# A three-stage network on one core: order of the second stage's vector work, the split of w_out2, and who copies the first block product out of PSUM

## The reference, cut to what matters

```python
# attention without softmax, 8 batches, 8 heads, seq 576, head size 64
kv = einsum('bhsd,bhse->bhde', k, v);  o = einsum('bhsd,bhde->bhse', q, kv)
x = o / sqrt(mean(o*o) + 1e-6) * g_norm                 # -> (8, 576, 512)
# first block
h = relu(x @ w_in);  u, v = h[..., :512], h[..., 512:]
v_n = (v - mean(v)) / sqrt(var(v) + 1e-6)
gated = u * (einsum('ts,bsd->btd', w_spatial, v_n) + b_spatial)
x = gated @ w_out
# second block
h = relu(x @ w_in2)                                      # (8, 576, 1024)
c = conv over seq, 3 taps per channel (conv_w), zero padding
out = (h * sigmoid(c)) @ w_out2                          # (8, 576, 512)
```

## Time and profile before

| | |
|---|---|
| median of 3 runs | 854.7 us |
| the profiled execution | 855.42 us, span 853.6 us, mean granted TensorE clock 0.992 |
| busy, share of span | PE 94%, PEld 82%, DVE 69%, ACT 49%, POOL 5% |
| phase 1, batch 3 | 47.04 us |
| phase 1, batches 1 and 2 together | 111.95 us |
| phase 2, an even and an odd batch | 49.25 and 55.15 us |

### The profile page before, as it was taken

One profiled execution on the slowest core, in us unless ns is written; L12 is line 12 of the kernel. 1 busy time (PEld: TensorE's weight loads), 2 busy tenths in 40 slices (PEclk: granted clock), 3 DMA queues, 4 the chain that ended last, 5 costly groups with the idle time before them and its releaser, 6 DMA issues. The chain is left out here.

```text
span 853.6 us, 15487 instructions
## 1 busy us (share of the span) xinstructions
PE 802.4 (94%) x5654; PEld 700.6 (82%) x5654; DVE 588.0 (69%) x1254; ACT 419.3 (49%) x753; POOL 40.1 (5%) x48
## 2 busy tenths in 40 slices
PE   8999969899999999999998998999899998998998
PEld 6679759598898979798996886978779687796976
DVE  3766555557667575758888788587876878669683
ACT  3664242433525262532636647365564555546563
POOL 4342020010000000000000000000000000000000
PEclk9999989989999999999999999999999999999999
DMA  9862615835435362222452120121210212102101
GB/s 311 276 230 57 238 76 169 298 86 223 148 98 182 78 240 70 83 57 98 164 228 98 50 95 31 35 97 50 98 50 12 97 49 97 49 13 97 49 1 61
DMA packets 35001, 96.86 MB, mean 113 GB/s; under 512 B 2738, under 2 KB 9106, under 8 KB 30228
## 3 DMA queue, kind: packets, MB, share of 16 engines
q1 hardware_dynamic: 33476, 90.09, 31.0%
q10 hardware_dynamic: 1488, 6.30, 2.0%
HBM read 66.11 MB, written 30.28 MB: 113 GB/s over the span
## 5 line engine op out<-in xcount | busy, mean ns | idle before, releaser
L627 PE MATMUL ps<-w_in_split,v_hg_split 128*128 128x512 f32 x832 | 209.6, 398 | 24.7 <-DVE v_hg_split L1295 17.4
L627 PEld LDWEIGHTS ps<-w_in_split,v_hg_split 128*128 128x128 f32 x832 | 151.4, 188 | 77.0 <-DVE v_hg_split L1295 38.9
L451 PE MATMUL ps<-w_sp_split,v_hg_split 128*128 128x288 f32 x896 | 120.4, 295 | 1.7 <-DVE w_sp_split L1121 1.3
L451 PEld LDWEIGHTS ps<-w_sp_split,v_hg_split 128*128 128x128 f32 x896 | 119.2, 188 | 2.1 <-issue 1.5
L451 PE MATMUL ps<-x_operand_split,w_in_split 128*128 128x288 f32 x768 | 105.5, 298 | 2.6 <-ACT work L709 2.6
L451 PEld LDWEIGHTS ps<-x_operand_split,w_in_split 128*128 128x128 f32 x768 | 103.1, 189 | 5.2 <-ACT work L709 3.3
L482 PE MATMUL ps<-w_in_split,x_operand_split 128*128 128x512 f32 x384 | 93.5, 396 | 0.0
L915 ACT ACTIVATE work<-work 128x576 f32<-128x576 f32 x64 | 44.0, 687 | 94.0 <-DVE work L1284 94.0
L482 PEld LDWEIGHTS ps<-w_in_split,x_operand_split 128*128 128x128 f32 x384 | 70.4, 188 | 20.9 <-issue 6.1
L1244 DVE TENSOR_TENSOR h_and_sums<-work,ps 128x288 f32<-128x288 f32 x64 | 27.5, 453 | 71.7 <-PE ps L619 39.4
L1244 DVE TENSOR_TENSOR h_and_sums<-h_and_sums,ps 128x288 f32<-128x288 f32 x160 | 67.1, 448 | 7.7 <-PE ps L619 7.4
(11 more groups left out here) (125 smaller groups left out, 1101.7 us busy)
## 6 DMA issues: line engine op xcount, KB each, us to landing
kv_raw<-kv_main_dram SPq DMA_DIRECT2D x8, 2048.0 KB, 10.2
q_raw<-q_T_dram SPq DMA_DIRECT2D x8, 1152.0 KB, 7.1
operand_scratch<-t_then_s SPq DMA_DIRECT2D x8, 1152.0 KB, 5.3
operand_raw<-operand_scratch SPq DMA_DIRECT2D x8, 1152.0 KB, 5.4
sq_then_r<-r_scratch SPq DMA_DIRECT2D x14, 576.0 KB, 6.0
operand_scratch<-work SPq DMA_DIRECT2D x24, 288.0 KB, 2.6
operand_more_raw<-operand_scratch SPq DMA_DIRECT2D x8, 864.0 KB, 7.1
w_out_split_scratch<-v_hg_split ACTq DMA_DIRECT2D x2, 2048.0 KB, 10.5
```

The costliest lines, as they stand in the source:

```text
L451: last = pe.matmul(pair[bank][:, c, :], st, mo[:, c * HALF:(c + 1) * HALF], start=(n == 0), stop=(n == len(steps) - 1))
L627: last = pe.matmul(PS[:, ROW_BANK[i], :], x, wout2[:, w, F_ORDER[e], :], start=(e == 0 and n == 0), stop=(e == FT - 1 and n == len(PASSES) ...
```

## The change

Five edits. (1) The storage order of the operand blocks is B11, B21, T2, T1, T3, T4, B22, so T1 comes with the first load. (2) The subtractions for w_out2 go from GpSimd to VectorE (`wo2_low`), and ScalarE's four copies go behind `v_hi(b, NT - 1)`. (3) `first_copy` goes from ScalarE to VectorE. (4) The lists of `body2` on ScalarE and VectorE get a new order; u2 may be written once sum 5 of the group before is done. (5) VectorE's bodies 1 and 2 of phase 1 are written out, and in batch 0 the subtraction for the bias row comes ahead of the last `v_lo`.

```diff
-B11, B21, T2, T3, T1, T4, B22 = range(7)
+B11, B21, T2, T1, T3, T4, B22 = range(7)
@@ gpsimd
-            for f in range(FT):
-                pool.wait_ge(s_wo2_hi, f + 1)
...
-                pool.tensor_tensor(wo2_lo[:, f % MT, :], ...ALU.subtract).then_inc(s_wo2, 1)
@@ scalar, body
-                        else:
-                            wo2_split(b - 1, i - 1)
...
                     v_hi(b, NT - 1)
+                    if isinstance(b, int) and b in (1, 2):
+                        for f in range(MT):
+                            wo2_split(b - 1, f)
                     u_relu(b, 2)
@@ scalar, body2: the new list
+ h_relu 0, tap1 0, h_relu 1, tap1 1, sigmoid 0, h_hi 0, h_relu 2, tap1 2, sigmoid 1,
+ h_relu 3, tap1 3, h_relu 4, h_hi 1, sigmoid 2, tap1 4, h_relu 5, h_hi 2, sigmoid 3,
+ tap1 5, h_relu 6, h_hi 3, sigmoid 4, tap1 6, h_relu 7, h_hi 4, sigmoid 5, operand 0,
+ tap1 7, operand 1, h_hi 5, sigmoid 6, operands 2 3, h_hi 6, sigmoid 7, operands 4-6, h_hi 7
@@ vector, body
+            def wo2_low(h, f):
+                dve.wait_ge(s_wo2_hi, h * MT + f + 1)
+                dve.tensor_tensor(wo2_lo[:, f, :], wo2_raw[:, f, :], wo2_hi[:, f, :].bitcast(F32), ALU.subtract).then_inc(s_wo2, 1)
...
-                v_lo(b, NT - 1)
                 if isinstance(b, int) and b == 0:
                     dve.wait_ge(s_b_hi, 1)
                     dve.tensor_tensor(wspB[96:97, :], ...)
+                v_lo(b, NT - 1)
+                if isinstance(b, int) and b in (1, 2):
+                    for f in range(MT):
+                        wo2_low(b - 1, f)
@@ vector, body2
+            def first_copy(b, g):
+                dve.wait_ge(s_in, b * PER_BATCH + g * NPROD + 1)
+                if g >= 2 or not (isinstance(b, int) and b == 0):
+                    own_sum(b, g, 2 - 2 * NPROD)
+                dve.tensor_copy(x1[g % 2], PS[:, g * NPROD % 8, 0:HALF]).then_inc(s_x1, 1)
@@ vector, body2: the new list (u2, c11, ... are the sums)
+ g0: copy u2 c11 u4 c12 u3 c22 c21, tap0 0
+ g1: copy, tap2 0, u2 c11, tap0 1, u4, mul 0, c12 u3, tap2 1, c22 c21
+ g2: copy, h_lo 0, u2 c11 u4, tap0 2, c12, mul 1, u3, tap2 2, c22 c21, h_lo 1
+ g3: copy, tap0 3, mul 2, u2, tap2 3, c11 u4, h_lo 2, tap0 4, c12, mul 3, u3, tap2 4,
+     c22 c21, h_lo 3
+ tap0 5, mul 4, tap2 5, tap0 6, h_lo 4, mul 5, tap2 6, tap0 7, h_lo 5, mul 6, tap2 7,
+ operand 0, h_lo 6, mul 7, operands 1 2, h_lo 7, operands 3-6
```

More of the change, by code:

```diff
@@ L939, in body2 @@
                 h_relu(b, 1)
[L940 removed]
                 tap1(b, 1)
                 sigmoid(b, 0)
+                h_hi(b, odd, 0)
                 h_relu(b, 2)
+                tap1(b, 2)
                 sigmoid(b, 1)
[L946 to L948 removed]
                 h_relu(b, 3)
                 tap1(b, 3)
+                h_relu(b, 4)
+                h_hi(b, odd, 1)
                 sigmoid(b, 2)
[L952 to L955 removed]
+                tap1(b, 4)
                 h_relu(b, 5)
[L957 removed]
+                h_hi(b, odd, 2)
                 sigmoid(b, 3)
+                tap1(b, 5)
                 h_relu(b, 6)
[L961 to L962 removed]
+                h_hi(b, odd, 3)
+                sigmoid(b, 4)
+                tap1(b, 6)
                 h_relu(b, 7)
[L964 to L966 removed]
+                h_hi(b, odd, 4)
                 sigmoid(b, 5)
[L968 removed]
+                if ahead:
+                    operand_hi(b + 1, 0)
                 tap1(b, 7)
+                if ahead:
+                    operand_hi(b + 1, 1)
+                h_hi(b, odd, 5)
                 sigmoid(b, 6)
[L971 removed]
+                if ahead:
+                    operand_hi(b + 1, 2)
+                    operand_hi(b + 1, 3)
+                h_hi(b, odd, 6)
                 sigmoid(b, 7)
                 if ahead:
[L974 to L978, removed]
+                    operand_hi(b + 1, 4)
+                    operand_hi(b + 1, 5)
+                    operand_hi(b + 1, 6)
                 h_hi(b, odd, 7)
[L980 to L982 removed]
                 for i in range(FULL):
@@ L1033, in inverse_root @@
                     dve.wait_ge(s_rP, MT)
-                if not isinstance(a, int):
+                if not isinstance(a, int) or a > 1:
                     dve.wait_ge(s_rst, (a - 1) * 4 * DMA)
@@ L1233, in _ @@
             body(0, True)
-            with dve.Fori(1, B - 1) as b:
+            body(1, True)
+            body(2, True)
+            with dve.Fori(3, B - 1) as b:
                 body(b, True)
@@ L1310, in body2 @@
                 sum_c21(b, 0)
-                sum_u2_c11(b, 1)
                 tap0(b, 0)
+                first_copy(b, 1)
+                tap2(b, 0)
+                sum_u2(b, 1)
+                sum_c11(b, 1)
+                tap0(b, 1)
                 sum_u4(b, 1)
-                tap2(b, 0)
+                mul(b, 0)
                 sum_c12(b, 1)
                 sum_u3(b, 1)
-                tap0(b, 1)
+                tap2(b, 1)
                 sum_c22(b, 1)
                 sum_c21(b, 1)
-                tap2(b, 1)
-                sum_u2_c11(b, 2)
-                mul(b, 0)
+                first_copy(b, 2)
+                h_lo(b, odd, 0)
+                sum_u2(b, 2)
+                sum_c11(b, 2)
                 sum_u4(b, 2)
@@ L1327, in body2 @@
                 sum_c12(b, 2)
+                mul(b, 1)
                 sum_u3(b, 2)
-                h_lo(b, odd, 0)
+                tap2(b, 2)
                 sum_c22(b, 2)
                 sum_c21(b, 2)
-                tap2(b, 2)
-                sum_u2_c11(b, 3)
-                mul(b, 1)
+                h_lo(b, odd, 1)
+                first_copy(b, 3)
+                tap0(b, 3)
+                mul(b, 2)
+                sum_u2(b, 3)
+                tap2(b, 3)
+                sum_c11(b, 3)
                 sum_u4(b, 3)
-                tap0(b, 3)
+                h_lo(b, odd, 2)
+                tap0(b, 4)
                 sum_c12(b, 3)
+                mul(b, 3)
                 sum_u3(b, 3)
-                h_lo(b, odd, 1)
+                tap2(b, 4)
                 sum_c22(b, 3)
                 sum_c21(b, 3)
[L1343 to L1350, removed]
+                h_lo(b, odd, 3)
+                tap0(b, 5)
+                mul(b, 4)
+                tap2(b, 5)
+                tap0(b, 6)
+                h_lo(b, odd, 4)
+                mul(b, 5)
+                tap2(b, 6)
+                tap0(b, 7)
+                h_lo(b, odd, 5)
+                mul(b, 6)
+                tap2(b, 7)
                 if ahead:
                     operand_lo(b + 1, 0)
-                h_lo(b, odd, FT - 2)
-                mul(b, FT - 1)
+                h_lo(b, odd, 6)
+                mul(b, 7)
                 if ahead:
@@ L1357, in body2 @@
                     operand_lo(b + 1, 2)
-                h_lo(b, odd, FT - 1)
+                h_lo(b, odd, 7)
                 if ahead:
-                    for k in range(3, NPROD):
-                        operand_lo(b + 1, k)
+                    operand_lo(b + 1, 3)
+                    operand_lo(b + 1, 4)
+                    operand_lo(b + 1, 5)
+                    operand_lo(b + 1, 6)
             for i in range(FT):
```

27 lines of the change are left out of this document (10 added, 17 removed).

## The result

The changed kernel takes 801.44 us (median of four runs, 799.78 to 803.28) against 854.89 (854.34 to 855.13) for the one before on the same chip: ratio 0.9376, 95% interval 0.9355 to 0.9397, 53.4 us less. The profiled execution took 801.49 us, with a span of 799.5 at a mean granted clock of 0.997.

A forecast was written before the change was run, and what follows sets the result against it. TensorE was taken to bound the kernel, losing time to the ordering of other engines' lists. 855.42 - 17.9 (w_out2) - 0.8 (bias row) - 36.4 (phase 2) = 800.3 us, median 0.7 lower: 799.6; range 796 to 814.

The forecast's parts named there:

- w_out2, -17.9 us: Phase 1, batches 1 and 2: moved splits no longer wait for w_out2's load, both batches take 47.04 us, 17.9 less.
- The cover: Phase 1: w_out2's copies and subtractions fit into ScalarE's and VectorE's waits, costing nothing; without it up to 9 us.
- Bias row, -0.8: Phase 1, batch 0: the earlier bias-row subtraction shortens TensorE's 1.28 us wait, saving 0.8 us.
- The copy's step, 0.37: Phase 2, VectorE: from a first copy's start to the next instruction takes 0.37 us, with ends 0.30 and 0.45.
- The replay of VectorE's list: Phase 2: walking VectorE's new list by measured steps; c11 starts at 22.1, rows at 22.7, even batch 44.65 us.
- Phase 2, -36.4: All eight batches of phase 2 take 381.2 us instead of 417.6, batch 0's rows starting 2.2 us later.
- no wait: Phase 2: TensorE's products 18 and 25 find their banks freed in time (12.5 before 14.4, 18.3 before 20.0).
- The list slips: Rival, chance 0.15: VectorE's list up to c11 runs longer, each microsecond costing 8 us in all; likely 812, at most 821.
- Rows keep VectorE's pace: Rival, chance 0.06: phase 2's rows start earlier but their products still wait for h_lo; 831 us.
- lockstep: Rival, chance 0.04: VectorE waits for ScalarE at each of phase 2's eight blocks, making the kernel slower; 863 us.
- w_out2 in the way: Rival, chance 0.08: w_out2's moved work delays phase 1's spatial products, 9 us more; 808.6 us.
- what is late next is c11: Phase 2: after the change, c11 of group 3 comes next as late, 22.7 against the products' end at 22.4.

The follow-up runs named there:

- e1: The kernel before with only phase 1's edits (w_out2 splits moved, subtractions on VectorE, bodies written out, bias row earlier), phase 2 as before: 836.49 us.
- e6: The changed kernel with u2 and c11 of group 3 ahead of tap0 3, mul 2 and tap2 3 in phase 2's batch 0 alone: 798.12 us.
- e4: The changed kernel with an extra VectorE copy of 256 PSUM columns ahead of each first copy: 809.95 us.
- e9: The changed kernel with the old storage order of the operand blocks and u2 waiting for sum 6 instead of 5: 801.60 us.
- e7: The changed kernel with w_out2's subtractions back on GpSimd, ScalarE's splits staying at their new place: 801.21 us.
- e2: The changed kernel with the first copy back on ScalarE, the new order of the lists kept: 796.73 us.
- e3: e1 with the first copy moved to VectorE ahead of u2 and c11, phase 2's lists otherwise in old order: 815.40 us.
- e5: e6 with c11 of group 3 also one place earlier, ahead of tap2 3, in all other batches of phase 2: 795.09 us.
- e11: e5 with e4's extra VectorE copy of 256 columns per group: 801.00 us.
- e10: e2 with u2 and c11 of group 3 ahead of tap0 3 in batch 0 of phase 2: 795.01 us.

## Why the prediction was right

The time forecast was 799.6 us and the one measured 801.4. The steps, one by one:

- **w_out2, -17.9 us: -17.96**, and e1 has the same two batches in 93.98 us (88.24 to 182.22). The cover was there. ScalarE and VectorE in batch 1 of the kernel after:

```profile
117.17 2.18 ACT L788 ACTIVATE v_hg_split<-w_out_raw 128x512 fp32r<-128x512 f32 x4
119.25 0.63 ACT L724 ACTIVATE work<-ps 128x576 f32<-128x576 f32 x1
120.87 0.65 ACT L724 ACTIVATE work<-ps 128x576 f32<-128x576 f32 x1 [0.99 <-PE ps L443]
```
```profile
118.00 2.50 DVE L1049 TENSOR_TENSOR v_hg_split<-w_out_raw,v_hg_split 128x512 fp32r<-128x512 f32 x4
124.65 0.76 DVE L1090 TENSOR_TENSOR work<-ps,work 128x576 f32<-128x576 f32 x1 [4.15 <-PE ps L443]
```

  The splits start at 117.17 without waiting for the load; the relu behind the pushed one still waits for TensorE (0.99 us left of the 2.53 in the earlier trace rows), and VectorE's gap ahead of the first gate still has 4.15 of 6.58 us.
- **Bias row, -0.8: -0.64.** The wait went from 1.28 to 0.64 us and is now ended by the last v_lo.
- **The copy's step, 0.37: 0.37.** The replay of VectorE's list held from batch 1 on: c11 starts 22.14 us into batch 2 (22.1), TensorE starts its rows at 22.72 (22.7), h_lo 7 ends at 40.02 (40.1) and the last operand split at 42.70 (42.7). An even batch took 44.61 us (44.65) and an odd one 50.07 (50.1). Batches 1 to 7 of phase 2 together, 334.3 us, are right to 0.1.
- **Phase 2, -36.4: -34.87.** The step that was mis-sized is batch 0: 46.85 us were forecast, 48.41 measured. Its rows started where they should, 437.61 - 412.66 = 24.95 us in (24.9), but the next batch began 23.46 us after them instead of 21.9. The windows of the kernel after around it show why: the gap, then the granted clock at 0.80, at 0.50 (one level, 1.2 GHz) and at 0.89, then full again.

```profile
435.74:437.61 1.87, 0.00 (x1) 0.03 (x1) 1.87 (x5) 1.27 (x2) 0.00 (x0) 1.00 0.25 38
437.61:440.00 2.39, 2.39 (x9) 1.92 (x10) 2.39 (x6) 1.29 (x3) 0.00 (x0) 0.80 0.95 348
440.00:442.00 2.00, 2.00 (x6) 1.63 (x5) 2.00 (x6) 1.59 (x3) 0.00 (x0) 0.50 1.05 412
442.00:444.00 2.00, 2.00 (x9) 1.61 (x8) 2.00 (x5) 1.38 (x3) 0.00 (x0) 0.89 0.49 175
444.00:461.07 17.07, 17.07 (x77) 14.11 (x76) 13.46 (x24) 10.84 (x18) 0.00 (x0) 1.00 0.01 5
```

  The prediction charged the gap for itself (2.2 us) and did not ask what the clock does after it, though the same had been read in phase 1. It is 1.56 us in this execution; not every execution has it (last section). With e6 the gap is gone, the granted clock stays at 1.00 and batch 0 takes 45.14 us: its rows start 2.0 us sooner and take 22.26. The prediction's "no wait" for TensorE's banks holds for the steady batches, not for batch 0, where a product of the kernel after starts 0.25 us late for its bank.

**The rivals.** *The list slips* did not come about, but its arithmetic is what e4 confirms: about a microsecond on VectorE in a batch is 7.6 us of span and 8.5 in the median. *Rows keep VectorE's pace* and *lockstep* are refuted by the group of 96 matmuls and by the table of VectorE's waits. *w_out2 in the way* is refuted by e1, where batches 1 and 2 take 93.98 us.

**What the prediction did not say.** It took the change as one thing and found it good. Read apart, T1's order and u2's wait are together worth 0 (e9), the choice of VectorE over GpSimd for w_out2 is worth 0 (e7), and the copy's move costs 4.7 us under the new order (e2 against after), while it gains 21.1 under the old one (e3 against e1). Both signs have one cause, what stands ahead of c11 of group 3. In the old order ScalarE's copy stood behind sigmoid and relu and VectorE stood idle for it, 1.71 us. In the new order ScalarE reaches the copy in time, and VectorE does not wait for it. c11 then ends at 22.22, just before it would hold TensorE; with the copies in VectorE's own list it ends at 22.59, too late by 0.33. The prediction named this ("what is late next is c11"), but 22.7 against 22.4 was not taken for a loss: it costs 44.61 - 44.20 = 0.41 us in an even batch. Batch 0 could be had 3.3 us shorter too (e6), of which 1.6 goes with the lower clock.

The prediction also set the prices of a PSUM copy on the two engines beside each other, from the Trainium skill, page "VectorE: DVE Perf Modes", section "The TRN2 errata": dearer on VectorE. The trace agrees in direction and not in figure: a copy of 288 columns takes 0.452 us on VectorE (line 1243), where the page's rule gives an estimate of 0.425, and 0.392 on ScalarE in the kernel before (line 932), against an estimate of 0.383. But the 4.7 us do not come from that difference of 0.06; they come from the path: in e5 the copy stays on VectorE, and with c11 early the time is 795.09.

The prediction quoted the same page's section "The DRAIN you can't avoid" in the Trainium skill by half. Its paragraph goes on that a next instruction which is not held starts earlier, and the trace agrees with that: 0.37 us from the start of a copy of 0.45 to the next instruction.

## What to carry to other kernels

An engine's instruction list can be replayed from the measured step of each instruction (its duration less the overlap with the next): 33 instructions between group 0 and c11 of group 3 came out right to 0.1 us. Do this for the list that releases the bound engine, count what stands ahead of the releasing instruction, and put that instruction early; which engine has a small operation matters only where that operation stands ahead of it. A replay has to ask for waits after every edit: in e2 the list was 1.1 us shorter and c11 only 0.37 sooner, since VectorE ran into TensorE's products. And price a gap in TensorE with what follows it, the restart and perhaps a stretch at a lower clock, not by its own length.

## What was not expected of the hardware

**A short gap costs more than it shows.** A gap of 0.17 us in an even batch of the kernel after costs 0.41 against e5, which has none (44.61 against 44.20); one of 0.38 in e11 costs 0.63. Two parts make this up. The first lies in how the gap is counted: it is shown from the modelled end of the last product, 0.96 us after its start, while a product without a wait hands over after 0.80. So a shown gap leaves out 0.16: 0.17 + 0.16 = 0.33 is the late start of the kernel after (22.72 against 22.39), and 0.38 + 0.16 that of e11 (22.94). The second part is 0.08 in the group of 96 matmuls behind it, 22.05 against 21.97 us. TensorE's weight loads for the first rows of batch 2, in e5 and in the kernel after:

```profile
529.61 1.48 PEld L619 LDWEIGHTS ps<-w_in_split,v_hg_split 128*128 128x128 f32 x7
```
```profile
533.86 1.22 PEld L619 LDWEIGHTS ps<-w_in_split,v_hg_split 128*128 128x128 f32 x6 [0.40 <-issue]
```

In e5 the first load starts 0.13 us ahead of the first rows matmul (529.74), in the kernel after at the same time as it. In e2 it is 0.04 ahead, no gap is shown, and the group has 22.05 too. So the longer group goes with a first weight load that had to wait; no run changes that alone, so it is not shown as the cause.

**The clock after a gap of some 1.9 us is not the same in every execution.** Ahead of batch 0's rows, 1.31 us (e2) were followed by 22.01 us for the 96 matmuls, 1.87 (after) by 23.63, 1.87 (e7) by 23.65 and 2.20 (e4) by 23.62. But e9 had a gap of 1.86 and then ran at full clock, in its timeline and window:

```profile
439.38 22.02 PE L619 MATMUL ps<-w_in_split,v_hg_split 128*128 128x512 f32 x96 [1.86 <-DVE h_and_sums L1234]
```
```profile
439.38:443.00 3.62, 3.62 (x16) 3.02 (x17) 3.62 (x8) 2.23 (x4) 0.00 (x0) 1.00 0.96 364
```

e9 paid elsewhere: in its start-up the granted clock was lower instead, as its windows show; in the kernel after the same two windows have 1.00.

```profile
10.00:20.00 10.00, 7.80 (x100) 6.67 (x99) 1.50 (x4) 1.36 (x3) 0.59 (x1) 0.89 1.02 350
20.00:30.00 10.00, 8.25 (x81) 5.35 (x82) 5.92 (x11) 7.07 (x15) 0.00 (x0) 0.94 1.05 402
```

So the profiled executions show two such places: batch 0, worth 1.6 us (after and e7), and the start-up, where phase 1's batch 0 begins 1.85 us later in e9 than in after and 2.5 later in e10. e2 and e5 met neither. That one execution can meet both is read from the times below, not from a trace. The mean granted clock of the timed executions goes with their times: after took 799.78 us at 1.000, 801.39 at 0.998, 801.49 at 0.997 and 803.28 at 0.996; e9 799.80 at 1.000, 801.33 and 801.60 at 0.998, 803.53 and 803.54 at 0.996. e5, whose batch 0 has no gap, took 795.02 to 795.37 at 0.999 to 1.000, and e10, without that gap too, 794.6 to 797.67, with the start-up of its profiled execution at 0.88. At full clock the change took 799.78 us, near the 799.6 of the forecast; its median has a place of lower clock in it, which the forecast lacks. What decides whether the clock falls after a gap is open. DMA traffic behind the gap of batch 0 was as high with the lower clock as without (shares of 0.95 and 0.96), so it does not tell them apart.
